# Copies of turned token blocks taken up in the fifth mixing step, half a u product held behind the first mixing product, block loads on other queues

## What is computed

```python
scores = q @ k.T / 8 + bias(distance, slope of the head)    # a local window of 96, 8 global keys
x = softmax(scores) @ v                                     # heads side by side: (2, 768, 512)
h = relu(x @ w_in); u, v = h[..., :512], h[..., 512:]       # w_in: 512 x 1024
v_n = layer_norm(v)                                         # over the 512 values
x2 = (u * (w_spatial @ v_n + b_spatial)) @ w_out            # w_spatial: 768 x 768, mixes tokens
t = x2 + (x2.T @ U @ V).T                                   # rank 32
out = t + relu(t @ w_ch1) @ w_ch2                           # 512 -> 2048 -> 512
```

## Time and profile before

| | us |
|---|---|
| three runs: median (lowest to highest) | 565.22 (563.82 to 565.73) |
| the profiled execution, its own time | 563.56 |
| its span, first to last instruction | 561.7 |
| TensorE busy | 525.1 (93%) |
| VectorE busy | 284.1 (51%) |
| ScalarE busy | 173.7 (31%) |
| POOL busy | 112.0 (20%) |

### The profile page before, as it was taken

One profiled execution on the slowest core, in us unless ns is written; L12 is line 12 of the kernel. 1 busy time (PEld: TensorE's weight loads), 2 busy tenths in 40 slices (PEclk: granted clock), 3 DMA queues, 4 the chain that ended last, 5 costly groups with the idle time before them and its releaser, 6 DMA issues.

```text
span 561.7 us, 7624 instructions
## 1 busy us (share of the span) xinstructions
PE 525.1 (93%) x2692; PEld 412.0 (73%) x2692; DVE 284.1 (51%) x797; ACT 173.7 (31%) x429; POOL 112.0 (20%) x136
## 2 busy tenths in 40 slices
PE   6799999999999999843999999999999999999996
PEld 5466666677777788632888888888888888888885
DVE  5879988877575368615622264614146424011112
ACT  4765666555554343203321011021111102011010
POOL 5833411100000002995049800000000000000000
PEclk9899999999999999885999999999999999999999
DMA  7979545551641122566013200002000002000002
GB/s 170 221 188 177 113 110 105 131 115 44 128 139 29 30 38 38 120 146 147 1 34 117 76 0 2 0 0 76 1 1 1 0 2 75 1 0 1 0 1 79
DMA packets 73739, 37.30 MB, mean 66 GB/s; under 512 B 58208, under 2 KB 68448, under 8 KB 73696
## 3 DMA queue, kind: packets, MB, share of 16 engines
q1 hardware_dynamic: 49776, 20.49, 17.1%
q0 software_dynamic: 3168, 11.54, 6.9%
q10 hardware_dynamic: 20752, 4.73, 4.2%
HBM read 32.54 MB, written 3.15 MB: 64 GB/s over the span
## 4 chain that ended last, share of the span: by engine, by line
PE 77%; DVE 8%; SPq 8%; issue 3%; DMA 2%; ACT 1%; ACTq 1%; POOL 0%; DVEq 0%
PE ps L1386 64%; SPq L460 7%; PE ps L1359 4%; PE ps L1403 4%; PE ps L1430 3%; DVE sc L1002 2%; DVE pr L1018 1%; PE ps L1531 1%; DMA qk_first<-in_k 1%; ACTq L637 1%; DVE q_turned L949 1%; PE ps L1363 1%; DVE small L1076 1%; DVE k_turned L949 0%; SPq L387 0%
## 5 line engine op out<-in xcount | busy, mean ns | idle before, releaser
L1307 DVE SCALAR_TENSOR_TENSOR hT_lo<-ps,hT_hi 128x512 fp32r<-128x512 f32 x48 | 33.2, 692 | 167.5 <-ACT hT_hi L868 167.5
L868 ACT ACTIVATE hT_hi<-ps 128x512 fp32r<-128x512 f32 x48 | 28.7, 598 | 223.2 <-PE ps L1386 223.2
L653 ACT ACTIVATE pr<-sc,small 128x256 f32<-128x256 f32 (+1 forms) x96 | 46.2, 483 | 46.6 <-DVE small L1002 46.4
L1002 DVE CUSTOM_DVE_ANT_0 sc<-ps,bias 128x256 f32<-128x256 f32 (+1 forms) x96 | 35.0, 398 | 14.4 <-PE ps L1403 12.2
L1386 PE MATMUL ps<-win_hi,xT_hi 128*128 128x512 f32 x96 | 39.8, 414 | 0.0
L1166 DVE STREAM_TRANSPOSE ys<-tokens 32x128 f32<-32x128 f32 x128 | 38.7, 302 | 1.8
L1386 PE MATMUL ps<-win_hi,xT_lo 128*128 128x512 f32 x96 | 37.7, 393 | 0.0
L1386 PE MATMUL ps<-win_lo,xT_hi 128*128 128x512 f32 x96 | 37.5, 391 | 0.0
L1386 PE MATMUL ps<-uT_hi,w1a_hi 128*128 128x512 f32 x96 | 37.5, 390 | 0.0
L1386 PE MATMUL ps<-uT_hi,w1a_lo 128*128 128x512 f32 x96 | 37.4, 389 | 0.0
L1386 PE MATMUL ps<-w2a_hi,hT_hi 128*128 128x512 f32 x96 | 37.3, 389 | 0.0
(11 more groups left out here) (165 smaller groups left out, 1083.1 us busy)
## 6 DMA issues: line engine op xcount, KB each, us to landing
w_raw<-in_moe_w_ch POOLq DMA_DIRECT2D x16, 512.0 KB, 4.3
vn<-in_v SPq DMA_DIRECT2D x12, 256.0 KB, 3.5
out<-ys SPq DMA_DIRECT2D x12, 256.0 KB, 2.2
qk_late<-in_q SPq DMA_DIRECT2D x24, 112.0 KB, 3.7
qk_late<-in_k SPq DMA_DIRECT2D x24, 112.0 KB, 3.8
wsp<-in_moe_w_spatial ACTq DMA_DIRECT2D x6, 384.0 KB, 4.4
vp<-in_v SPq DMA_DIRECT2D x10, 224.0 KB, 4.3
w_raw<-in_moe_w_in POOLq DMA_DIRECT2D x4, 512.0 KB, 5.1
```

Of the source, the lines that this page charges most:

```text
L653: act.activation(pr[:, k % 3, e, 0:w], sc[:, k % 2, e, 0:w], ACT.Exp, bias=nmax[:, k % 2, e:e + 1], scale=-1.0, accum_out=sums[:, k % 3, e ...
L868: act.activation(hT[0][:, n % 2, :], h1_ps(n), ACT.Relu).then_inc(s["hT_hi"], 1)
L1002: dve.tensor_tensor_reduce(out=sc[:, k % 2, e, 0:w], in0=scores_ps(k, e)[:, 0:w], in1=bias[:, 2 * p + e, WINDOW - w:WINDOW], scale=-SCALE, ...
L1307: dve.scalar_tensor_tensor(hT[1][:, n % 2, :], h1_ps(n), 0.0, hT[0][:, n % 2, :], ALU.max, ALU.subtract).then_inc(s["hT_lo"], 1)
```

## The change

In `products(1)`, `uT_hi(0, j)` and `uT_lo(0, j)` for all j go to step 4 (NT - 2). `turn_rows` starts one tile earlier, and its last call stands behind `gv_lo(1, 5)`. The last half of the u product of tile (1, 5), HELD, is issued behind `mix_tokens(1, 0)`. `load_blocks(0)` is now `load_rows(0)` on POOL's queue, with its own semaphore `blocks_first`; `load_blocks(4)` and `(5)` stand behind gT_hi. The diff, without the branch `every`, which this input doesn't take:

```diff
+HELD = B - 1, NT - 1, 3
@@ gpsimd
+            def load_rows(t):
+                for y in range(TURNS):
+                    pool.dma_start(wsp_blocks(t)[y * TURN:(y + 1) * TURN, :, :, :].rearrange("p a k c -> p (a k) c"),
+                                   blocks_d[t, y, :, :, :]).then_inc(s["blocks_first"], 16)
...
             pool.wait_ge(s["v4_split"], PIECES)
+            wait(pool, "wsp_transposed", 2 * NT)
+            load_rows(0)
             wait(pool, "qk_turned", TILES)
             for n in (ready["out"], ready["out"] + 1):
                 load_chunk(n)
@@ scalar, products
-                    if b:
-                        load_blocks(t + 4)
-                    elif t + 2 < NT:
+                    if b == 0 and t + 2 < NT:
                         load_wsp(t + 2)
                     if t:
                         x2_hi(b, t - 1, True)
                     gT_hi(b, t)
-                    if b and t < TB:
-                        uT_hi(0, t)
+                    if b:
+                        load_blocks(t + 4)
+                    if b and t == NT - 2:
+                        for j in range(TB):
+                            uT_hi(0, j)
@@ scalar, window
                     if t + 2 < NT:
                         load_wsp(t + 2)
-                    elif t + 2 == NT:
-                        load_blocks(0)
@@ vector, turn_wsp
-                dve.wait_ge(s[f"blocks_loaded{t % 2}"], 16 * TURNS * (t // 2 + 1))
+                if t:
+                    dve.wait_ge(s[f"blocks_loaded{t % 2}"], 16 * TURNS * ((t + 1) // 2))
+                else:
+                    dve.wait_ge(s["blocks_first"], 16 * TURNS)
@@ vector, products
-                    if b and 0 < t <= TB:
-                        uT_lo(0, t - 1)
                     if t:
                         x2_lo(b, t - 1, True)
                     gT_lo(b, t)
+                    if b and t == NT - 2:
+                        for j in range(TB):
+                            uT_lo(0, j)
@@ vector, window
                     layer_norm(1, t)
-                    if 2 <= t:
-                        turn_rows(t - 2)
+                    if t < TB:
+                        turn_rows(t - 1)
...
                 gv_lo(1, NT - 1)
+                turn_rows(TB - 1)
@@ tensor, u_v_late
                 for q in (2, 3):
-                    if t != NT - 2:
+                    if t != NT - 2 and (b, t, q) != HELD:
                         u_v_piece(b, t, q, wide)
@@ tensor, products
                     mix_tokens(b, t, True)
+                    if b and t == 0:
+                        u_v_piece(*HELD, True)
```

More of the change, by code:

```diff
@@ L334, in program @@
         s = {n: ctx.enter_context(nc.semaphore(n)) for n in """
-            n_loaded q_loaded0 q_loaded1 k_loaded0 k_loaded1 v_loaded0 v_loaded1 wsp_loaded blocks_loaded0 blocks_loaded1 chunk_loaded0 chunk_loaded1 u_loaded bsp_loaded
+            n_loaded q_loaded0 q_loaded1 k_loaded0 k_loaded1 v_loaded0 v_loaded1 wsp_loaded blocks_first blocks_loaded0 blocks_loaded1 chunk_loaded0 chunk_loaded1 u_loaded bsp_loaded
             v4_loaded stored0 stored1 stored2 stored3 iota_ready ident_ready setup_step dense_ready waited slopes
@@ L781, in every @@
                         v4_hi()
-                    if b:
-                        load_blocks(0)
-                    else:
+                    if b == 0:
                         load_wsp(0)
@@ L1222, in every @@
                         layer_norm(b, t)
-                        if b and t < TB:
+                        if b and t < TB - 1:
                             turn_rows(t)
                     gv_lo(b, NT - 1)
+                    if b:
+                        turn_rows(TB - 1)
                     if b == 0:
```

## The result

The changed kernel takes 541.08 us in the median (539.97 to 542.04, 4 runs), against 565.48 us for the kernel before in the same runs. The ratio is 0.957 with a 95% interval of 0.954 to 0.960: 24.4 us faster, 540.6 were forecast. The profiled execution of the changed kernel took 542.04 us (span 540.2), 1.0 us more than its median; that of the kernel before took 563.56 (span 561.7), 1.9 less than its own. The two spans are only 21.5 us apart, and it is these 21.5 us that the traces can follow.

A forecast was written before the change was run, and what follows sets the result against it. Outside TensorE's empty stretches, back-to-back matrix products bound the kernel. Closing the mixing hole (22.66 us) and the block-load waits (1.9) takes 24.6 us off the 565.22 us median: 540.6 us, range 538.5 to 545.5.

The forecast's parts named there:

- The signs: Traces would show no long TensorE wait, full clock, uT_hi waiting for gT, copies 42 us from about 205, gv_lo near 0.7.
- No TensorE wait over 0.5 us: Between 180 us and hidden(0), which was to start near 266, TensorE would never wait longer than 0.5 us.
- rival (a): All TensorE waits between 180 us and hidden(0) go, as summed: 539.5 to 542 us, chance 0.76.
- The stall of 17.23 us and its clock: Batch 1's mixing: TensorE's x_lo wait, from late copies, and low clock go; full-speed pieces sum to 42.82 us against 65.48.
- Copies: 64 x 0.663 us: SyncE's queue: 64 issues at 0.663 us each, from 207.0 to 249.4 us, landed by 251.7, 8.4 us before needed.
- Cost 0 to 0.3 ... I take 0: POOL's splits beside mixing steps 0 to 5 may hold uT_lo in step 4 and delay gated by 0 to 0.3 us.
- rival (b): POOL beside the mixing holds uT_lo in step 4: 6 us lost, 546.6, or 543 to 545 with fewer held; chance 0.14.
- can be held as well, and has the 3.6 us until its product to spare: VectorE's wsp_lo, reading two SBUF inputs, may be held by POOL but has 3.6 us until its TensorE product.
- The held half: Start of batch 1's mixing: 1.36 us of product fills the 0.85 gated(0) wait; gv_lo(1, 5) wait, 0.87, goes too.
- Block loads on POOL: Step 5 of batch 0: TensorE's waits of 0.38 and 1.52 us go, gain 1.9; four issues cost 2.3 to 12.4.
- load_blocks(4) and (5) behind gT_hi and x2_hi: Batch 1's mixing on ScalarE: load_blocks(4) issued about 231.5 to 234.6 us, landed by 238, turned behind gate(2) at 241: hidden.
- The sum: 22.66 us from the mixing plus 1.9 from the block loads make 24.6 us, for a median of 540.6 us.

The follow-up runs named there:

- e5: Changed kernel with POOL's subtraction for the first eight chunks replaced by filling with zeros, that work left out: 539.95 us, 0.9516 of the kernel before.
- e8: Changed kernel with POOL's subtraction for the first eight chunks cut into four pieces of 256 columns: 539.06 us, 0.9507 of the kernel before.
- e9: Changed kernel with POOL's subtraction in quarters and the second half of wspT_lo behind the next gate: 540.04 us, 0.9527 of the kernel before.
- e6: Changed kernel with SyncE's 64 copies held back until the first mixing product of batch 1 is done: 550.17 us, 0.9695 of the kernel before.
- e1: Kernel before with only uT_hi and uT_lo in step 4 and the new places of turn_rows: 550.23 us, ratio 0.9692.
- e11: Changed kernel with POOL's subtraction in quarters and the half product not held: 540.96 us, 0.9553 of the kernel before.
- e0: Changed kernel again, unaltered: 541.94 us, 0.9559 of the kernel before; B, from first mixing product to hidden(0) without the held half's 1.36 us, was 44.83 us.
- e3: Changed kernel with the last half of tile (1, 5)'s u product not held, back in front of the mixing: 541.25 us, 0.9553 of the kernel before.
- e7: Changed kernel with turn_rows at its old places in VectorE's order: 541.91 us, 0.9554 of the kernel before.
- e10: Kernel before with only the block loads of tile 0 moved from ScalarE's to POOL's queue: 563.75 us, ratio 0.9946.
- e2: Changed kernel with the four block loads of tile 0 back on ScalarE's queue: 546.2 us, 0.9622 of the kernel before.

## Why the prediction was right, step by step

- **The signs.** Of those that were to show it right, uT_hi's place, the copies, gv_lo (0.69 us) and the clock (1.00 from 172 us to hidden(0)) came as said. "No TensorE wait over 0.5 us" did not: there are two, 0.62 and 1.33, and hidden(0) starts at 268.98 us instead of near 266. The time lies where rival (a), "all waits go", has it, but not all waits went.
- **The stall of 17.23 us and its clock.** Right in mechanism and size. e5, e8 and e9 reach 42.71 us where the sum of pieces said 42.82. e6 brings the stall back by lateness alone. e1 shows that the copies' move carries most of the gain, 16.4 us.
- **Copies: 64 x 0.663 us.** 41.96 us from 205.83, 42.4 from about 205 forecast; in the other traces with the earlier start they took up to 44.6 us (e11), still in time.
- **"Cost 0 to 0.3 ... I take 0" for POOL beside the mixing.** This is the step that failed. In kind it is rival (b), which had 0.14, but that was placed at uT_lo and priced at 2.4 to 6 us. The term measured 2.1 to 2.4 us (B of e0 and of the changed kernel less 42.71). I had seen that wspT_lo "can be held as well, and has the 3.6 us until its product to spare", and had looked at TensorE's product as the one that waits. Behind the held pair on VectorE stands the next gate, and the pair (4.4 us), what comes before it and the gate together outlast the time that TensorE has from one gate_transpose to the next. uT_lo was stretched too (four took 3.70 us) and cost nothing, as I had it. The Trainium skill (SBUF — State Buffer, "Who interferes with whom"), which I had named, says just what e5 and e8 show: two SBUF inputs on VectorE against an operation of GpSimd that reads SBUF. By that rule every wspT_lo in these steps was at risk, and I worked it out for uT_lo alone. The trace also has the other side: gT_lo, which reads ps and only one tile of SBUF, took its 0.69 us at 230.12, in the middle of a subtraction of POOL (229.31 to 231.71).
- **The held half.** I credited it with the waits for gv_lo and for gated(0), with the clock behind them. The wait for gated(0) is right (0.84 us in e3, 0.85 in e11). For that for gv_lo either the held half or the moved turn_rows is enough (e3, e7). And it is not free: it put POOL in a worse phase, so that in this kernel it gains nothing measurable (0.9553 without, 0.9559 with). The clock was no fixed price even before the change: in e10, where both waits stand (0.87 and 0.84 us), it stayed at 1.00 behind them.
- **Block loads on POOL.** 1.9 us forecast, 2.0 in the two traces, but 2.0 to 4.2 in e10's runs: the hole also lets the clock fall in some executions (e1, e2), which the profiled one of before didn't show. I had priced clock only where I saw it. Four issues took 2.91 us, near the low one of my bounds (2.3 to 12.4). From the Trainium skill (SBUF — State Buffer, "The 'DVE blocks DMA' trap (SWDGE)", with the figures in the section behind it, "A bandwidth-pool intuition that's wrong") I had an estimate of 12.4. These runs don't test it: the issues ran from 176.16 to 179.07, and VectorE's fp32 operations from SBUF to SBUF, its scaling of the probabilities, at 174.51 and 180.46, outside that stretch.
- **load_blocks(4) and (5) behind gT_hi and x2_hi.** "Hidden", I wrote. In the changed kernel that is so; left where they were, they cost 1.18 and 1.35 us in e1, and the first of them 1.07 in e10.
- **The sum.** 24.6 us forecast, 24.4 measured, and that is partly luck: POOL took 2.1 to 2.4 us off, and about as much came back from a side that I had left out. The 2 us between medians and traces are open. The clock lost behind the hole at 181 to 184 us is a candidate, argued from e1, e2 and e10 and not shown; clock lost behind the two waits at 229 and 231 us, which differs between the traces of before and of e10, can't be excluded as another.

## What to carry to other kernels

When a stall goes, take each engine's queue over the stretch again, in order, and ask of every instruction that another engine can hold what stands behind it on its own engine. The late one was not the consumer of the held data but the next instruction in the queue. Cut what holds into pieces, or put what is awaited in front of what may be held: each gave about 2 us here. And price a wait of TensorE with its clock even if the one profile at hand shows none.

## What the runs showed of the hardware that I had not expected

- What holds VectorE is measured here by one operation at a time: a wspT_lo (two SBUF inputs) takes 0.52 to 0.55 us by itself, 1.42 and 1.73 beside a cast of POOL of 1.05 us (e5, changed kernel), 2.74 beside a subtraction of 2.59 us, and each ends 0.4 us after POOL's operation. Beside POOL's filling with zeros it took 0.54 (e5).
- Nearly the same waits can leave the granted clock alone or not. At 181 to 185 us, 0.38 and 1.52 us left it at 1.00 in the profile of before; 0.98 and 1.52 in e1 and 0.69 and 1.52 in e2 brought it to 0.57 and 0.69 in 184 to 188 us. At the first mixing step, 0.87 and 0.85 us brought it to 0.57 in 231 to 235 us in the kernel before, and 0.87 and 0.84 us left it at 1.00 in e10; so did a single wait of 0.84 or 0.85 in e3 and e11.
- A load of 96 KB in runs of 128 bytes is not the same on the two kinds of queue. With four of them moved, ScalarE's queue q10 lost 3,136 packets (20,752 to 17,616, 784 each) and POOL's q0 gained 192 (3,168 to 3,360, 48 each). The issue cost 0.73 us on POOL and 0.78 on ScalarE, and the loads land in 3.1 and 3.3 us, so my bound of 3.1 us an issue, by packets, rested on the wrong count.
